# A gated-attention and two-expert kernel: new engine orders at the change from attention to the experts, and POOL's steps moved in the first iterations

## The reference

```python
# attention: batch 2, 8 heads, 768 steps, head size 40
m_new = np.maximum(f_gate[:, :, t] + m, i_gate[:, :, t])
f_stab, i_stab = np.exp(f_gate[:, :, t] + m - m_new), np.exp(i_gate[:, :, t] - m_new)
C = f_stab * C + i_stab * np.einsum('bhd,bhe->bhde', vt, kt)
n = f_stab * n + i_stab * kt
y_t = sigmoid(o_gate_t) * (C q_t) / max(|n . q_t|, 1)
# first expert: x is 1536 x 320, w_in 320 x 2048
h = x @ w_in
P = a[0] + a[1] * h + a[2] * h * h + a[3] * h * h * h
Q = 1.0 + |b[0]| * |h| + |b[1]| * h * h
x = (P / (Q + 1e-06)) @ w_out
# second expert: rms norm, w_gate and w_val 320 x 1536
xn = x / sqrt(mean(x * x) + 1e-06) * rms_g
out = (silu(xn @ w_gate) * (xn @ w_val)) @ w_out
```

## Time and profile before

| what | value |
|---|---|
| three timed runs | 469.82, 473.56, 478.21 us |
| profiled execution | 468.82 us |
| its span | 467.0 us |
| granted TensorE clock | 1.00 of full speed throughout |
| busy: PE, DVE, ACT, POOL | 455.5, 328.5, 289.4, 250.6 us |
| ACT: absolute L819, linear L828, slope L836 | 0.60, 0.68, 1.24 us |
| ACT: log_q L841, inverse L852, high L858 | 1.15, 1.03, 1.05 us |
| POOL: one half of denominator L589, low L595 | 1.30, 1.31 us |
| POOL: split_main1 L518, low_out1 L622 | 1.28, 1.56 us |
| DVE: numerator_1 L1203, numerator_2 L1208, lo_of_x L1196 | 0.74, 0.74, 0.56 us |
| DVE: newton_1 L1213, newton_2 L1218, quotient L1223 | 1.28, 1.23, 1.27 us |

### The profile page before, as it was taken

How to read it: one execution, slowest core, us unless ns; L and a number is a source line. 1 busy time by engine, 2 the same in 40 slices (tenths; PEclk the granted TensorE clock), 3 DMA queues, 4 the chain that set the end, 5 groups by cost and what they waited for, 6 DMA issues and landing times.

```text
span 467.0 us, 7429 instructions
## 1 busy us (share of the span) xinstructions
PE 455.5 (98%) x2679; PEld 398.8 (85%) x2680; DVE 328.5 (70%) x462; ACT 289.4 (62%) x468; POOL 250.6 (54%) x271
## 2 busy tenths in 40 slices
PE   8999999988999999999999999999999999999997
PEld 4888997866999888998899888888888888888886
DVE  7999997998899998999999543484343444534333
ACT  6788887799889999999988648532111222211111
POOL 4476698858898897988989555981000000000000
PEclk9999999999999999999999999999999999999999
DMA  8998930230000000000005030000010000100001
GB/s 245 332 317 267 268 92 1 91 135 1 0 1 1 1 1 1 0 1 0 2 0 214 2 135 3 0 1 0 1 56 1 0 0 1 44 14 1 1 0 58
DMA packets 8372, 26.78 MB, mean 57 GB/s; under 512 B 1216, under 2 KB 3136, under 8 KB 7824
## 3 DMA queue, kind: packets, MB, share of 16 engines
q1 hardware_dynamic: 8336, 26.30, 17.6%
HBM read 24.33 MB, written 1.97 MB: 56 GB/s over the span
## 4 chain that ended last, share of the span: by engine, by line
PE 82%; DVE 5%; ACT 3%; issue 2%; POOL 1%; DVEq 0%; POOLq 0%; ACTq 0%
PE ps L1620 7%; PE ps L1621 7%; PE ps L1622 7%; PE ps L1550 6%; PE ps L1552 6%; PE ps L1551 6%; PE ps L1568 4%; PE ps L1569 4%; PE ps L1570 4%; PE ps L1528 4%; PE ps L1526 4%; PE ps L1527 4%; PE ps L1624 3%; PE ps L1625 3%; PE ps L1474 2%; PE ps L1529 2%
## 5 line engine op out<-in xcount | busy, mean ns | idle before, releaser
L992 ACT ACTIVATE ab<-ps 128x512 f32<-128x512 f32 x36 | 21.6, 599 | 117.6 <-PE ps L1625 117.6
L1337 DVE TENSOR_TENSOR ab<-ps,ab 128x512 f32<-128x512 f32 x36 | 24.9, 691 | 84.7 <-ACT ab L992 84.7
L589 POOL TENSOR_TENSOR qq<-qq,ab 128x512 f32<-128x512 f32 x48 | 61.2, 1296 | 20.9 <-ACT qq L836 20.8
L595 POOL TENSOR_TENSOR g_lo<-cc,g_hi 128x512 fp32r<-128x512 f32 x48 | 61.9, 1310 | 6.0 <-ACT g_hi L858 6.0
L1550 PE MATMUL ps<-wo_hi,g_hi 128*128 128x320 f32 x192 | 59.9, 312 | 2.1 <-POOL g_lo L595 1.1
L1552 PE MATMUL ps<-wo_hi,g_lo 128*128 128x320 f32 x192 | 59.3, 309 | 0.0
L1551 PE MATMUL ps<-wo_lo,g_hi 128*128 128x320 f32 x192 | 59.3, 309 | 0.0
L1568 PE MATMUL ps<-wo_hi,g_hi 128*128 128x320 f32 x136 | 42.0, 309 | 0.2 <-ACT g_hi L1000 0.2
L1570 PE MATMUL ps<-wo_hi,g_lo 128*128 128x320 f32 x136 | 42.0, 309 | 0.0
L1569 PE MATMUL ps<-wo_lo,g_hi 128*128 128x320 f32 x136 | 42.0, 309 | 0.0
L1550 PEld LDWEIGHTS ps<-wo_hi,g_hi 128*128 128x128 f32 x192 | 36.0, 188 | 5.7 <-issue 2.6
(11 more groups left out here) (189 smaller groups left out, 1252.5 us busy)
## 6 DMA issues: line engine op xcount, KB each, us to landing
qk<-q_k_dram SPq DMA_DIRECT2D x12, 448.0 KB, 9.0
wo_raw<-w_out_dram SPq DMA_DIRECT2D x7, 640.0 KB, 7.0
kv<-kv_n_dram SPq DMA_DIRECT2D x10, 372.0 KB, 6.9
w_raw<-w_main_dram SPq DMA_DIRECT2D x4, 512.0 KB, 7.7
out_dram<-y_out SPq DMA_DIRECT2D x12, 160.0 KB, 1.9
w2c_raw<-w_main_dram SPq DMA_DIRECT2D x1, 1536.0 KB, 6.2
sig_o<-o_n_dram SPq DMA_DIRECT2D x1, 1280.0 KB, 7.7
rest_raw<-w_rest_dram SPq DMA_DIRECT2D x2, 512.0 KB, 7.6
```

What stands on the lines that cost most here:

```text
L589: pool.tensor_tensor(qq[m % 2][:, h, :], qq[m % 2][:, h, :], ab[m % 2][:, h, :], ALU.mult)\
L595: pool.tensor_tensor(glo(n), cc[n // 2 % CR][:, n % 2, :], ghi(n).bitcast(F32), ALU.subtract)\
```

## The change

Five parts, all in the orders of instructions.

1. GpSimd's first iterations: `input_steps(1)` stands ahead of `ones(2)`, and GpSimd waits for VectorE's third `spread_whole` ahead of `split_main1(0)`.
2. `gate_columns` uses transposes (one pass through TensorE) in place of float32 matmuls by the identity.
3. TensorE's order from iteration 10 to `second(4)`, and the places of the zeros.
4. GpSimd's, ACT's and VectorE's orders over the same stretch.
5. `high(0)` on ACT waits in addition for the last hU.

```diff
@@ gpsimd
-            for it in range(NT - 1):
+            for it in range(NT - 2):
                 if it == 2:
                     low_of_b(1)
+                if it == 0:
+                    input_steps(1)
                 if it + 2 < NT:
                     ones(it + 2)
-                if it == 0:
-                    input_steps(1)
...
                 if it == 3:
+                    pool.wait_ge(whole_spread, B + 1)
                     split_main1(0)
...
-                elif it == 9:
-                    split_rest1(2)
-                elif it == 10:
-                    split_main1(5)
-                    low_out1(3)
+            split_main1(5)
+            split_rest1(2)
+            low_out1(3)
+            gated(NT - 3)
             denominator(0)
-            low_out1(4)
+            normalised(NT - 3)
             split_main1(6)
...
             low(1)
-            split_main1(7)
             denominator(3)
             low(2)
+            split_main1(7)
+            low_out1(4)
             low(3)
@@ scalar
             def high(m):
                 act.wait_ge(g_done, m + 1)
+                if m == 0:
+                    act.wait_ge(hu_done, NT)
...
             absolute(0)
             linear(0)
-            hi_of_x(NT - 5)
             absolute(1)
+            slope(0)
+            round_out1(5)
             linear(1)
-            slope(0)
             hi_of_x(NT - 4)
-            round_out1(5)
-            round_main1(7)
             log_q(0)
             inverse(0)
             absolute(2)
             linear(2)
             absolute(3)
+            slope(1)
             linear(3)
-            slope(1)
+            absolute(4)
             hi_of_x(NT - 3)
-            absolute(4)
             linear(4)
             log_q(1)
+            high(0)
             inverse(1)
+            absolute(5)
             hi_of_x(NT - 2)
-            high(0)
-            absolute(5)
+            slope(2)
             linear(5)
-            slope(2)
+            hi_of_x(NT - 1)
+            round_main1(7)
             absolute(6)
+            absolute(7)
             linear(6)
-            hi_of_x(NT - 1)
-            absolute(7)
             linear(7)
+            log_q(2)
+            slope(3)
+            inverse(2)
             high(1)
-            log_q(2)
-            inverse(2)
-            slope(3)
             round_out1(6)
-            for k in range(4, NP):
+            log_q(3)
+            absolute(8)
+            linear(8)
+            absolute(9)
+            inverse(3)
+            slope(4)
+            linear(9)
+            high(2)
+            round_out1(7)
@@ vector
-            for it in range(NT - 2):
+            for it in range(NT - 3):
...
+            carried(NT - 3)
+            probs(NT - 2)
+            state(NT - 3)
+            lo_of_x(NT - 6)
+            combine(NT - 3)
+            denominators(NT - 3)
+            lo_of_x(NT - 5)
             numerator_1(0)
-            lo_of_x(NT - 5)
             numerator_2(0)
             probs(NT - 1)
             carried(NT - 2)
-            lo_of_x(NT - 4)
             numerator_1(1)
             combine(NT - 2)
+            lo_of_x(NT - 4)
             carried(NT - 1)
             numerator_2(1)
             denominators(NT - 2)
             newton_1(0)
+            newton_2(0)
             numerator_1(2)
-            newton_2(0)
+            quotient(0)
             numerator_1(3)
+            numerator_2(2)
             combine(NT - 1)
-            quotient(0)
-            lo_of_x(NT - 3)
-            numerator_2(2)
             numerator_2(3)
             denominators(NT - 1)
+            lo_of_x(NT - 3)
             numerator_1(4)
             newton_1(1)
             numerator_2(4)
-            lo_of_x(NT - 2)
             newton_2(1)
             numerator_1(5)
+            lo_of_x(NT - 2)
             numerator_2(5)
+            quotient(1)
             lo_of_x(NT - 1)
-            quotient(1)
             numerator_1(6)
+            numerator_1(7)
             numerator_2(6)
-            numerator_1(7)
             numerator_2(7)
...
@@ tensor
-                    mm = pe.matmul(ps[:, 7, at_:at_ + BH], cumA[:, c * L:(c + 1) * L], ident[0:BH, 0:BH],
-                                   start=True, stop=True)
+                    mm = pe.transpose(ps[:, 7, at_:at_ + BH], cumA[:, c * L:(c + 1) * L], ident[0:BH, 0:BH])
...
                     if n == 0 and t == 1:
-                        add_zeros(0, 5)
+                        add_zeros(0, 8)
+                    if n == 0 and t == 2:
+                        add_zeros(0, 4)
...
+            causal(NT - 2)
+            log_weights(NT - 2)
+            carry(NT - 3)
+            scores(NT - 2)
+            updates(NT - 3)
+            transposes(NT - 6)
+            intra(NT - 3)
             causal(NT - 1)
+            transposes(NT - 5)
             log_weights(NT - 1)
             first(0)
-            transposes(NT - 5)
             first(1)
...
             first(2)
             first(3)
+            first(4)
+            transposes(NT - 3)
             intra(NT - 1)
-            transposes(NT - 3)
-            first(4)
             first(5)
...
             second(0)
-            add_zeros(0, 6)
-            for n in (8, 10):
-                first(n)
-                first(n + 1)
-                second(n - LAG1)
-                second(n - LAG1 + 1)
+            second(1)
+            first(8)
+            first(9)
+            second(2)
+            first(10)
+            second(3)
+            first(11)
+            second(4)
```

More of the change, by code:

```diff
@@ L877, in _ @@
             weights(0)
-            for it in range(NT - 1):
-                if it == NT - 2:
-                    round_main1(6)
-                    round_rest1(3)
+            for it in range(NT - 3):
                 if it == 0:
@@ L913, in _ @@
                     round_out1(3)
-                elif it == 9:
-                    round_main1(5)
-                    round_out1(4)
-                if 3 <= it < NT - 2:
+                if 3 <= it:
                     hi_of_x(it - 3)
+            weights(NT - 2)
+            spread(NT - 1)
+            hi_of_x(NT - 6)
+            round_out1(4)
+            round_rest1(3)
+            round_main1(5)
+            hi_of_x(NT - 5)
+            weights(NT - 1)
+            round_main1(6)
             absolute(0)
             linear(0)
-            hi_of_x(NT - 5)
             absolute(1)
+            slope(0)
+            round_out1(5)
             linear(1)
-            slope(0)
             hi_of_x(NT - 4)
-            round_out1(5)
-            round_main1(7)
             log_q(0)
@@ L967, in _ @@
                     high(k - 2)
-                if k == 4:
-                    round_out1(7)
                 if k in (PB + 4, PB + 5):
@@ L1257, in _ @@
                     gate_steps(1)
-                if it == NT - 3:
-                    state(it)
                 combine(it)
@@ L1263, in _ @@
                 denominators(it)
-                if it < NT - 3:
-                    state(it)
+                state(it)
                 if it == 0:
@@ L1644, in _ @@
             updates(0)
-            for it in range(1, NT - 2):
+            for it in range(1, NT - 3):
                 if it >= 2:
@@ L1676, in _ @@
             first(6)
+            transposes(NT - 1)
             first(7)
-            transposes(NT - 1)
             second(0)
-            add_zeros(0, 6)
-            for n in (8, 10):
-                first(n)
-                first(n + 1)
-                second(n - LAG1)
-                second(n - LAG1 + 1)
+            second(1)
[6 more added lines that the diff above has]
+            second(4)
             for n in range(LAG1 + 5, NB * FT1 + LAG1):
```

1 line of the change is left out of this document (added).

## The result

The changed kernel took 464.36 us in the median of five runs (464.22, 464.17, 475.69, 466.05, 464.36). The kernel before, timed beside it in five runs, had its median at 473.56 us (469.82 to 478.21). The ratio is 0.985, with a 95% interval of 0.980 to 0.990. The interval leaves out the slow runs, so the run of 475.69 us, at a mean granted clock of 0.971, is not in it; by the two medians the ratio would be 0.981. The forecast was 468.4 us in a range of 462.8 to 475.7, and "within 2%". Both hold.

The account below looks back on a forecast made before the run. TensorE was taken as the bound, with time to win only in its waits in the first iterations and the change-over: 1.0 + 4.2 = 5.2 us off the 473.56 median gives 468.4 us, range 462.8 to 475.7.

Parts of the forecast that it names:

- The first term, 0.6 us for hU: First iterations: L1054 on VectorE ends about 1 us sooner, of which TensorE, waiting for hU, can use 0.59 us.
- The second term, 0.9 us for L1104 and L518: First iterations: with GpSimd waiting before L518, VectorE's L1104 falls from 2.14 to 1.23 us, saving 0.9 us.
- The give-back of 0.5 us: First iterations: the moved L518 locks VectorE's tiny L1180, so 0.95 of 1.5 us reach TensorE.
- The early sum: First iterations: 0.6 + 0.9 - 0.5 = 1.0 us, with bounds of 0 and 1.5.
- The columns at nothing: Gate columns as transposes save 0.5 us on TensorE, but its next wait, for VectorE's L1104, covers this: counts nothing.
- The change-over, 4.2 us: From attention to the first expert: first(12) starts at 115.1 instead of 119.34, the sum 1.76 + 1.2 + 1.2.
- The term of slope(3), 1.2 + 1.2 us: Change-over: slope(3) sooner on ACT removes TensorE's waits at second(2) and first(11), 1.2 us each.
- The term for second(1) ahead of first(8), 1.76 us: Change-over: second(1) replaces TensorE's zeros and waiting; first(8) begins at the same 102.0, so 1.76 us are won.
- GpSimd's margins: Change-over: low(2) is done 1.35 us and low(3) 0.75 us before TensorE wants them.
- GpSimd as the bound: Rival, change-over: GpSimd becomes the bound, a gain of 0.6 instead of 4.2 us, time 472.0; chance 0.15.
- That the early part gives nothing: Rival, first iterations: TensorE's input after L1104 is late for another reason, such as loads; time 469.4; chance 0.12.
- ACT held at high(0): Rival, change-over: high(0) waits for a late last hU and stops ACT; at worst about 475.7 us; chance 0.08.

Follow-up runs that it names:

- early_steps: The kernel before with `input_steps(1)` alone moved ahead of `ones(2)` on GpSimd: 469.44 us in one run, against 471.01 for the kernel before beside it.
- early_all: The kernel before with the three early edits alone (`input_steps(1)`, GpSimd's wait, transposes for the gate columns): 472.68 us, ratio 0.998.
- slope_back: The changed kernel with ACT's old order: high(1) ahead of log_q(2), slope(3) behind inverse(2): 475.48 us in one run, mean clock 0.978.
- second_back: The changed kernel with second(1) behind first(9) again and six zeros ahead of first(8) on TensorE: 465.17 us in one run.
- splits_back: The changed kernel with both weight splits ahead of denominator(3) on GpSimd again: 464.63 us in one run.
- after: The changed kernel's first profiled execution, 464.22 us; the median of its five timed runs was 464.36 us.
- after_again: The changed kernel run once more, nothing altered: 464.75 us, ratio 0.988.
- xlo_first: The changed kernel with the last x_lo ahead of quotient(1) on VectorE: 465.01 us, ratio 0.989.
- late_all: The changed kernel with the three early edits undone, only the new orders from iteration 9 on: 467.72 us, ratio 0.993.
- early_columns: The kernel before with transposes for `gate_columns` alone: 479.56 us in one run, mean clock 0.975.
- early_wait: The kernel before with GpSimd's wait for the third `spread_whole` ahead of L518 alone: 472.71 us in one run.

## Why the prediction was right, step by step

1. **Where time can be won: right.** Behind first(12) the two kernels agree within 0.07 us.
2. **The first term, 0.6 us for hU: too small here, and it has no fixed size.** In the changed kernel VectorE carries the whole 1.07 us that L1066 gained, and it is VectorE that TensorE waits for at L1116. The forecast counted what TensorE could use at once and forgot that the next wait is VectorE's. But VectorE keeps it only where its instruction on `wv` (L1132, now L1144) doesn't meet GpSimd's L569. In early_steps it did, and 0.6 us of the 1.07 were gone; the forecast has no term for this meeting. Against this, TensorE's first fourteen warm-up matmuls took 6.14 us instead of 4.92 in the execution of the changed kernel, and VectorE's L1066 stood 0.38 us later on the clock. All fourteen start 0.43 us apart there; before, the spacing goes from 0.43 to 0.22 us behind the ninth. That looks like half clock, though the profile's figure for the clock is 1.00 in both.
3. **The second term, 0.9 us for L1104 and L518: 0.39.** L1104 (now L1116) gave 0.39 us, because L569 met it in this execution. Where the load came by 31.2 us, as in early_all, slope_back, second_back and splits_back, it took 1.22 as forecast. The forecast had taken it that nothing behind GpSimd's new wait matters; it didn't look at what stands ahead of it, a load and the work behind that load.
4. **The give-back of 0.5 us: mechanism right, not met here.** In this execution it cost nothing. Where L518 followed the spread copy at once, it cost 0.7 us (0.87 or 0.88 against 0.17).
5. **The early sum**: 1.07 + 0.39 - 0.38 = 1.08, against 1.10 read at the transposes and 1.0 forecast. The sum agrees better than its terms, and that is luck: it hangs on the landing of a load. In the five executions at full clock with all early edits (after, after_again, xlo_first, second_back, splits_back) the transposes start at 37.35, 37.33, 37.39, 37.94 and 36.81 us, so the early part is worth 0.5 to 1.6 us. In second_back `wv` took 1.03 us and the tiny instruction 0.88; in splits_back neither was held, nor was the spread copy.
6. **The columns at nothing: right.** The wait behind them took them up.
7. **The change-over, 4.2 us: 3.67.** In the old clock (1.1 us added) second(0) ended at 100.61 against 100.3, second(2) started at 106.10 against 105.8, first(11) at 111.98 against 111.45, first(12) at 115.67 against 115.1. Half of the miss is there at second(0). Its chain starts at first(3), which TensorE ended near 85.4 in the old clock and not at 84.95; x_lo(11) ended 0.3 us late at the other end of the chain. The rest is the wait before first(11), 0.34 us where 0.1 was forecast.
8. **Its parts.** The term of slope(3), 1.2 + 1.2 us, measured 1.96 when slope(3) and high(1) were put back. The term for second(1) ahead of first(8), 1.76 us, was mis-sized as a price of that swap: undone alone it cost 1.13 us at second(2) and 0.55 us at first(12). The forecast let first(8) start at the same time with the swap and without it. In fact it starts 0.72 us later with it (63.92 against 63.20 us behind the transposes): 0.36 us are VectorE's new order, which the forecast laid to the swap, and about as much is the late second(0). What is left at second(2) ends for its half in the wait at first(11). The two measured parts make 2.5 of the 3.67 us. The remaining 1.2 us, with the rest of VectorE's, ACT's and TensorE's new orders, were not taken apart, and parts that overlap needn't add up to the whole.
9. **GpSimd's margins: right.** Low(2) had 1.37 us in hand (forecast 1.35), low(3) 0.68 (0.75).

**Rivals.** GpSimd as the bound fell in splits_back. That the early part gives nothing is not excluded by the times (early_all 0.998, 0.993 to 1.004), but the traces show 0.5 to 1.6 us where all early edits are in and the clock is full, and 0.39 in early_steps. The loads that the rival names do set this size. ACT held at high(0) did not occur: hU was ready at 89.12, and high(0) started at 89.98 right behind log_q(1). The cover was 0.9 us, where 1.2 was forecast.

**Why 464.4 and not 468.4.** The mechanisms gave 4.7 us between two profiled executions near full clock, against 5.2 forecast. The medians lie 9.2 us apart. Most of the difference is the clock of the runs: of 19 later runs of the kernel before, 15 had a mean clock under 0.996 (for the five of the first result it isn't on record), and four of five of the changed one had 0.996 or more. The last section has the numbers. So that the time came out 4 us under the forecast is nothing that the forecast's mechanism gave. I had subtracted a gain from a median that held such stretches, as if the changed kernel would have as many. Whether the early edits make them rarer, or the five runs were lucky, stays open: runs with a mean clock of at least 0.996 were 4 of 19 for the kernel before, 4 of 10 for early_all, 4 of 10 for late_all and 8 of 9 for the changed kernel.

## What to carry to other kernels

Where one engine is the bound, walk its waits one by one, and follow each to the engine that is late; a saving on that engine can count in full at its next meeting, also where the bound engine can't use it at once. But lay the shifted instructions of VectorE beside those of GpSimd first: a shift of 1 us can bring two together that had missed each other, and then 0.6 us of it are gone. When two edits serve the same wait, price them together and not by their parts, since the second finds the wait already shortened. Before a gain is subtracted from a median, read the granted clock of the runs: what they lose there can be more than the change is worth.

## What was not expected of the hardware

TensorE's granted clock fell from full speed to half, from 2.4 to 1.2 GHz, for 3 to 24 us in all, somewhere between 25 and 60 us, in five of the ten profiled experiments. Two of them by stretch, first late_all, then early_all (from:to, length, busy by engine, clock, DMA):

```profile
20.00:26.00 6.00, 6.00 (x56) 5.31 (x55) 5.71 (x10) 4.53 (x12) 4.84 (x5) 1.00 1.01 379
26.00:31.00 5.00, 5.00 (x30) 4.61 (x29) 4.17 (x11) 1.67 (x7) 2.25 (x4) 0.66 1.03 307
```

```profile
30.00:36.00 6.00, 4.42 (x38) 3.82 (x35) 5.77 (x8) 4.74 (x5) 3.57 (x6) 1.00 1.03 281
36.00:46.00 10.00, 10.00 (x54) 9.35 (x53) 6.42 (x16) 5.07 (x12) 4.78 (x8) 0.50 0.57 156
```

In late_all TensorE was busy for all 6.00 us before the clock fell; in early_all it had waited 1.57 us for the spread copy just ahead. So a wait of TensorE may go before the fall, but no wait has to stand right ahead of it. At half clock TensorE did 54 instructions in 10 us where it does 97 from 36 to 46 us in the trace before. What the clock costs was fitted over 19 runs of the kernel before: the span is 466.2 us at full clock, and 4.5 us longer for each 0.01 that its mean is lower (465.4 us at 0.999, 480.4 us at 0.968). Put to full clock by that, the means are 466.2 us for the kernel before, 465.8 for early_all, 462.9 for late_all, 461.6 and 462.3 for the changed one, and 461.4 for xlo_first, each uncertain by 0.2 to 0.4 us. At equal clock the change is thus worth about 4.3 us, or 0.9% (3.9 us by the runs of the changed kernel that stood beside the 19): 3.3 to 3.7 us from the change-over and 0.4 to 1 from the early part. What makes the clock fall wasn't found.

A load that GpSimd waits for (the memset L502 of iteration 4) was followed by that memset at 29.7 to 32.0 us in the twelve profiled executions, with no relation to their order: 29.70 us in early_columns, 29.93 in early_steps, 31.21 in late_all, 32.02 in xlo_first. Which of GpSimd's instructions stands beside which of VectorE's in the early part follows from it.

What such a meeting costs can be told to a few hundredths of a microsecond. These VectorE instructions have two inputs in SBUF. Where one of them started while a product or difference on GpSimd had more than 0.14 us to go, it ended at a fixed time behind the end of GpSimd's instruction (the `den` and `wv` of iteration 4, the `a_step` of the second segment):

| VectorE instruction | free | ends behind GpSimd's by | executions |
|---|---|---|---|
| spread copy, L1104 (64x1024) | 1.22 us | 1.07 to 1.08 us | 7 |
| `a_step`, L1054 (16x512) | 0.67 us | 0.55 us | 3 |
| `wv`, L1132 (128x328) | 0.49 us | 0.35 to 0.36 us | 7 |
| `den`, L1180 (128x8) | 0.17 us | 0.03 us | 4 |

Each is 0.12 to 0.14 us less than the instruction takes when free. In four executions (early_wait, early_all, late_all, slope_back) `wv` met the decay of C (L512) and L569 right behind it, and waited for both: it took 1.49 to 1.67 us.
